# Weight splitting in the second layer of a float32 attention and two-MoE kernel: high parts in two pieces, low parts of five groups on VectorE

## The chip, the cores and the metric

One core of one Trainium2 chip runs the whole kernel. The metric is the device time of one execution in microseconds (us), median of three runs; lower is better. The engines are called TensorE (PE in rows), VectorE (DVE), ScalarE (ACT), GpSimd (POOL) and SyncE (SP), which here only issues DMAs.

## What is computed

The delta-rule attention of 32 heads (4 x 8, 768 steps, head size 48) gives a 3072 x 384 matrix, and two dense layers follow. Only the second of them is touched:

```python
def _moe2_ref(x, w_in, w_out):
    h = x @ w_in                 # 3072 x 384 by 384 x 2048
    r = np.maximum(h, 0.0)
    g = r * r
    return (g @ w_out)           # 2048 x 384
```

## The kernel before

**Precision.** TensorE multiplies numbers of the reduced type float32r. Each float32 tensor is split: the *high* part is a copy by ScalarE that is rounded to float32r, the *low* part is the tensor less its high part. A product takes three matmuls: high by high, high by low, low by high. One matmul here has a 128x128 weight and 512 moving columns; three of them are called a *triple* below.

**Quads.** The second layer works on a pair of 512-token tiles and a group of 256 hidden features (two blocks of 128) at a time. The 2 x 2 result blocks of that *quad* are made with 11 combined products instead of 12 (u, w, c11 twice, t twice, c00, c10 twice, c01 twice), on sums and differences of weights and tokens that are made ahead. There are 3 token pairs and NG = 8 weight groups, so 24 quads: q = 8 * pair + g. The four result blocks b = 0 to 3 pass through ScalarE (relu), VectorE (square), ScalarE (high part, `block_high`) and VectorE (low part, `block_low`), and are then multiplied by `w_out` (`block_output(q, b, kt)`, 12 triples). In TensorE's program the output triples of quad q-1 stand between the products of quad q: 11 + 12 = 23 triples to a quad. Only two PSUM banks hold the products: bank 0 takes u, then c11 on top, then c00, then c01; bank 1 takes w, t, c10. So u of the next quad waits until VectorE has read c01 (`c01_ready`), c11 waits until ScalarE has copied u to `part_u` (`u_part_ready`), t waits for VectorE's `part_w`, c10 for `part_t`, c01 for VectorE's reading of c00.

**Weights of the second layer.** For each group g SyncE loads `w_in` in two DMAs and `w_out` in one into a staging place (`x2_raw` for g from 2 on), GpSimd makes the combinations (`combine_weights`, six instructions), ScalarE makes the high parts (`high_weights`, one instruction of 1280 columns for the `w_in` side, one of 768 for the `w_out` side) and GpSimd the low parts (`low_weights`, 1280 and 768 columns). The load of g+1 waits for both low parts of g, since there is one staging place. Groups 0 to 2 are made during the last tile of the first layer, groups 3 to 7 during quads 0, 1, 2, 4 and 5. Group g is first multiplied in quad g. After group 7, `load_raw(1)` brings the next token pair to the same place, and GpSimd makes five sums (`x2_sums`) and nine low parts (`x2_lows`) of it, ScalarE the nine high parts (`x2_part`), before quad 8; the same again before quad 16.

**What sets the order.** Every engine runs its own program strictly in the written order; semaphores join them. `drain(NTT - 1)` is the copy of the first layer's last accumulators to `y_out`, three ScalarE instructions in quad 0; output triples of block 1 of quad 0 write these accumulators, so they wait for it.

## Time and profile before

| | |
|---|---|
| median of 3 runs | 976.04 us (975.87 to 976.7) |
| the profiled execution | 977.68 us, span of its instructions 975.9 us |
| mean granted TensorE clock | 0.985 |
| TensorE matmul busy | 948.2 us (97%) |
| VectorE busy | 673.8 us (69%) |
| ScalarE busy | 453.9 us (47%) |
| GpSimd busy | 172.4 us (18%) |

Busy shares are unions over the span. Matmuls overlap in the records: one of 512 columns is shown as 0.39 us long, but a new one starts every 0.23 us when nothing holds TensorE up, so a stall is seen in the distance between two starts. The second layer begins at 575.7 us of the span and lasts to its end.

### The profile page before, as it was taken

How to read it: one execution, taken by the hardware profiler on the slowest of the kernel's cores; microseconds unless marked ns; L12 is line 12 of the kernel's file. 1: busy time of each engine (PE TensorE's matmuls, PEld its weight loads, DVE VectorE, ACT ScalarE, POOL GpSimd, SP SyncE). 2: the span in 40 equal slices, each digit the busy share in tenths (PEclk: the TensorE clock that was granted, in tenths of full speed). 3: DMA queues.
4: the chain of work that ended last, by engine and by line, in shares of the span. 5: the costliest groups of instructions: out<-in, count | busy, mean ns of one | idle time of the engine just before them, and what ended most of it. 6: DMA issues, size and time to landing. Idle time of an engine off the chain costs nothing.

```text
span 975.9 us, 23047 instructions
## 1 busy us (share of the span) xinstructions
PE 948.2 (97%) x9448; PEld 767.1 (79%) x9448; DVE 673.8 (69%) x1566; ACT 453.9 (47%) x768; POOL 172.4 (18%) x165
## 2 busy tenths in 40 slices
PE   7899999999999999999999997999999999999997
PEld 6688788778877877787778885787888888888886
DVE  7799798687978788889644545666565564756553
ACT  6667443553355435444545534443453334534333
POOL 5810000000000000000008833543530101400000
PEclk7899999999999999999999998999999999999999
DMA  8252240112012201110013111112002000010001
GB/s 259 83 174 66 60 131 35 34 41 81 35 34 85 69 11 34 48 56 1 2 40 132 52 38 71 39 38 74 29 33 97 1 1 1 6 59 1 1 1 65
DMA packets 31015, 51.71 MB, mean 53 GB/s; under 512 B 2496, under 2 KB 19904, under 8 KB 30912
## 3 DMA queue, kind: packets, MB, share of 16 engines
q1 hardware_dynamic: 30912, 50.24, 15.6%
q8 instruction: 76, 1.25, 0.5%
q14 instruction: 27, 0.22, 0.1%
HBM read 40.80 MB, written 9.44 MB: 51 GB/s over the span
## 4 chain that ended last, share of the span: by engine, by line
PE 83%; DVE 7%; ACT 6%; issue 2%; DMA 2%; SPq 1%; ACTq 0%; DVEq 0%
PE psum L1649 19%; PE psum L1579 18%; PE psum L1569 17%; PE psum L1550 17%; PE psum L1300 2%; PE psum L1386 2%; PE psum L1325 1%; PE psum L1437 1%; DVE act_g L1988 1%; ACT kn_sb L950 1%; PE psum L1444 1%; DMA ring<-in_v_s 1%; PE psum L1251 1%; PE psum L1469 1%; DVE act_g L2032 1%
## 5 line engine op out<-in xcount | busy, mean ns | idle before, releaser
L1579 PE MATMUL psum<-x_high,w 128*128 128x512 f32 x528 | 191.8, 393 | 9.0 <-DVE act_g L2067 6.1
L1569 PE MATMUL psum<-g_hi,w 128*128 128x512 f32 x576 | 197.6, 398 | 0.0
L1550 PE MATMUL psum<-x_hi,w 128*128 128x512 f32 x576 | 197.5, 398 | 0.0
L2032 DVE TENSOR_TENSOR act_g<-act_g 128x512 f32<-128x512 f32 x96 | 75.2, 783 | 82.3 <-ACT act_g L1143 59.1
L1550 PEld LDWEIGHTS psum<-x_hi,w 128*128 128x128 f32 x576 | 108.0, 188 | 26.5
L1569 PEld LDWEIGHTS psum<-g_hi,w 128*128 128x128 f32 x576 | 108.0, 188 | 26.0 <-issue 1.8
L1579 PEld LDWEIGHTS psum<-x_high,w 128*128 128x128 f32 x528 | 100.2, 190 | 31.9 <-issue 10.0
L1569 PE MATMUL psum<-g_lo,w 128*128 128x512 f32 x288 | 112.3, 390 | 0.0
L1550 PE MATMUL psum<-x_lo,w 128*128 128x512 f32 x288 | 111.9, 390 | 0.0
L1046 ACT ACTIVATE act_g<-act_g,half 128x512 f32<-128x512 f32 x86 | 62.2, 723 | 105.3 <-DVE act_g L1984 104.9
L1988 DVE TENSOR_TENSOR act_g<-act_g,psum 128x512 f32<-128x512 f32 x96 | 65.7, 684 | 61.3 <-ACT act_g L1046 57.5
L1649 PE MATMUL psum<-quad_hi,w 128*128 128x512 f32 x288 | 105.6, 396 | 0.0
L1649 PE MATMUL psum<-g_hi,w 128*128 128x512 f32 x288 | 103.8, 389 | 0.0
L1579 PE MATMUL psum<-x_low,w 128*128 128x512 f32 x264 | 103.6, 392 | 0.0
L1054 ACT ACTIVATE g_hi<-act_g 128x512 fp32r<-128x512 f32 x96 | 60.7, 632 | 89.1 <-DVE act_g L1988 60.9
L1993 DVE TENSOR_TENSOR g_lo<-act_g,g_hi 128x512 fp32r<-128x512 f32 x96 | 68.0, 708 | 24.1 <-ACT g_hi L1054 23.0
L1984 DVE TENSOR_SCALAR act_g<-psum 128x512 f32<-128x512 f32 x86 | 58.9, 685 | 21.8 <-PE psum L1550 21.4
L1085 ACT ACTIVATE act_g<-act_g 128x512 f32<-128x512 f32 x72 | 45.6, 633 | 61.1 <-DVE act_g L2058 60.7
L798 POOL TENSOR_TENSOR x_sum<-x_raw 128x512 f32<-128x512 f32 x15 | 20.9, 1412 | 249.6 <-DMA x_raw<-between_layers 162.2
L1649 PEld LDWEIGHTS psum<-quad_hi,w 128*128 128x128 f32 x288 | 55.0, 191 | 12.0 <-issue 0.4
L1649 PEld LDWEIGHTS psum<-g_hi,w 128*128 128x128 f32 x288 | 54.1, 188 | 11.3
L1847 DVE TENSOR_TENSOR x_inv<-x_inv,tmp 128x126 f32<-128x126 f32 (+35 forms) x305 | 62.5, 245 | 0.2
(188 smaller groups left out, 1492.3 us busy)
## 6 DMA issues: line engine op xcount, KB each, us to landing
kt_sb<-in_k_t SPq DMA_DIRECT2D x24, 256.0 KB, 4.1
qt_sb<-in_q_t SPq DMA_DIRECT2D x23, 256.0 KB, 3.4
ring<-in_v_s SPq DMA_DIRECT2D x24, 192.0 KB, 3.1
between_layers<-y_out SPq DMA_DIRECT2D x6, 768.0 KB, 3.5
x_raw<-between_layers SPq DMA_DIRECT2D x6, 768.0 KB, 5.6
gram_or_states<-in_k_s SPq DMA_DIRECT2D x15, 192.0 KB, 2.4
x_raw<-in_w_in SPq DMA_DIRECT2D x6, 384.0 KB, 3.0
x_raw<-in_w_out SPq DMA_DIRECT2D x6, 384.0 KB, 4.1
```

The source lines that it names most:

```text
L1046: act.activation(act_g[n % 2][:, :], act_g[n % 2][:, :], ACT.Square, bias=half[:, 0:1], scale=0.5).then_inc(m_ready, 1)
L1054: act.activation(g_hi[n % 2][:, :], act_g[n % 2][:, :], ACT.Copy).then_inc(g_hi_ready, 1)
L1085: act.activation(quad_act(b)[:, :], quad_act(b)[:, :], ACT.Relu).then_inc(relu_ready, 1)
L1550: ins = pe.matmul(h_ps[n % 2][:, :], w_in_part(f // GW, part)[:, kt, fs], x[:, kt, :], start=(at == 0), stop=(at == len(terms) - 1))
L1569: ins = pe.matmul(acc_ps[0][kt][:, :], w_out_part(f // GW, part)[:, f % GW, ds], g[n % 2][:, :], start=(f == 0 and j == 0), stop=(f == NF ...
L1579: ins = pe.matmul(bank[at][:, :], weight[:, part, w * P:(w + 1) * P], moving[:, x, :], start=(first and c == 0 and j == 0), stop=(c == len ...
L1649: ins = pe.matmul(acc2_of(pair, token_of(b))[kt][:, :], w2[g][:, part, at:at + P], moving[b][:, :], start=(g == 0 and b < 2 and j == 0), s ...
L1847: dve.tensor_tensor(x_inv[:, odd:j + 1:2, j + 1:BLK], x_inv[:, odd:j + 1:2, j + 1:BLK], outer[odd], ALU.add).then_inc(inv_chain, 1)
L1984: dve.tensor_scalar(act_g[n % 2][:, :], h_ps[n % 2][:, :], -1.0, 1.0, ALU.max, ALU.min).then_inc(a_ready, 1)
L1988: dve.tensor_tensor(act_g[n % 2][:, :], act_g[n % 2][:, :], h_ps[n % 2][:, :], ALU.max).then_inc(g_act_ready, 1)
L1993: dve.tensor_tensor(g_lo[n % 2][:, :], act_g[n % 2][:, :], g_hi[n % 2][:, :].bitcast(F32), ALU.subtract).then_inc(g_lo_ready, 1)
L2032: dve.tensor_tensor(quad_act(b)[:, :], quad_act(b)[:, :], quad_act(b)[:, :], ALU.mult).then_inc(square_ready, 1)
```

## The change

The high parts of groups 3 to 7 are no longer made at one place: the 1280-column piece follows `block_high(q, 0)` in quads 0 to 4, the 768-column piece `block_high(q, 1)`. Their low parts are subtracted by VectorE at the end of its quad, groups 3 to 7 in quads 0 to 4; GpSimd keeps groups 0 to 2 and makes only the combinations of the others. The load of `w_in` of the next group no longer waits for the `w_out` side, which has a semaphore of its own. VectorE reads c01 before it squares block 2. TensorE makes one output triple of the old quad before u. `drain(NTT - 1)` moves from behind relu of block 0 to behind `block_high(0, 2)`. The sums for quad 8 each wait for a step of quad 6 or 7.

```diff
             def load_weights2(g):
...
                 elif g:
-                    sp.wait_ge(w2_lo_ready, 2 * g)
+                    sp.wait_ge(w2_lo_ready, 2 * g - 1)
...
+                if g:
+                    sp.wait_ge(w2_lo_ready, 2 * g if g != 2 else 2)
                 sp.dma_start(plain_out(g), w_out2.rearrange("(f p) n -> p f n", p=P)[:, g * GW:(g + 1) * GW, :]
-                             ).then_inc(w2_loaded[at], 16)
+                             ).then_inc(w2_out_loaded[at], 16)
...
                     if pair > 1:
                         pool.wait_ge(w_part_ready, NG * (pair - 1) + i + 3)
+                    elif pair and i == 2:
+                        pool.wait_ge(c01_ready, NG - 1)
+                    elif pair:
+                        pool.wait_ge(w_part_ready, NG - 1 if i < 2 else NG)
...
-            for g in range(1, NG):
+            for g in range(1, EARLY2):
                 combine_weights(g)
                 low_weights(g)
+            for g in range(EARLY2, NG):
+                combine_weights(g)
...
                 act.activation(quad_act(0)[:, :], bank[0][:, :], ACT.Relu).then_inc(relu_ready, 1)
-                if q == 0:
-                    drain(NTT - 1)
                 block_high(q, 0)
...
-                if q in (0, 4):
-                    high_weights(6 if q else 3)
+                if q < NG - EARLY2:
+                    high_weights_in(q + EARLY2)
                 act.wait_ge(c00_ready, q + 1)
                 block_relu(1)
...
                 block_high(q, 1)
-                if q == 5:
-                    high_weights(7)
+                if q < NG - EARLY2:
+                    high_weights_out(q + EARLY2)
...
-                if q == 1:
-                    high_weights(4)
+                if q == 0:
+                    drain(NTT - 1)
                 act.wait_ge(c01_ready, q + 1)
                 block_relu(3)
...
-                if q == 2:
-                    high_weights(5)
...
             def quad(q):
+                block_output(q - 1, 0, 0)
                 if q > 1:
                     u_product(q)
-                block_output(q - 1, 0, 0)
                 block_output(q - 1, 0, 1)
+                if q > 1:
+                    w_product(q)
+                block_output(q - 1, 0, 2)
...
+            def low_weights(g):
+
+                for out_part, cols in enumerate((slice(0, IN_COLS), slice(IN_COLS, ALL_COLS))):
+                    dve.wait_ge(w2_hi_ready, 2 * g + out_part + 1)
+                    dve.wait_ge(w2_lo_ready, 2 * g + out_part)
+                    dve.tensor_tensor(w2[g][:, LOW, cols], staged2(g)[:, cols], w2[g][:, HIGH, cols].bitcast(F32),
+                                      ALU.subtract).then_inc(w2_lo_ready, 1)
...
                 block_low(q, 1)
-                block_square(q, 2)
                 dve.wait_ge(c01_done, q + 1)
                 dve.wait_ge(quad_lo_ready, blocks_by(q, 1))
                 dve.tensor_tensor(quad_act(3)[:, :], part_w[:, :], bank[0][:, :], ALU.subtract).then_inc(c01_ready, 1)
+                block_square(q, 2)
                 block_low(q, 2)
                 block_square(q, 3)
+                if q < NG - EARLY2:
+                    low_weights(q + EARLY2)
```

**VectorE, from the reading of c10 in quad 0 to `part_w` of quad 1.** Line 2062 (later 2090) reads c10, 2067 (2094) reads c01, 2032 (2060) squares, 2037 (2065) is `block_low`, where `g_lo0` and `g_lo1` are blocks 2 and 3, and 2046 (2074) is `part_w`. Before:

```order
L2062 TENSOR_TENSOR act_g0<-part_w,psum 128x512 [waits quad_lo_ready,c10_done]
L2037 TENSOR_TENSOR quad_lo1<-act_g1,quad_hi1 128x512 [waits quad_hi_ready]
L2032 TENSOR_TENSOR act_g0<-act_g0 128x512 [waits relu_ready]
L2067 TENSOR_TENSOR act_g1<-part_w,psum 128x512 [waits quad_lo_ready,c01_done]
L2037 TENSOR_TENSOR g_lo0<-act_g0,g_hi0 128x512 [waits quad_hi_ready]
L2032 TENSOR_TENSOR act_g1<-act_g1 128x512 [waits relu_ready]
L2037 TENSOR_TENSOR g_lo1<-act_g1,g_hi1 128x512 [waits quad_hi_ready]
L2046 TENSOR_TENSOR part_w<-psum,part_u 128x512 [waits c01_ready,u_part_ready,w_done]
```

The same place in the change:

```order
L2090 TENSOR_TENSOR act_g0<-part_w,psum 128x512 [waits quad_lo_ready,c10_done]
L2065 TENSOR_TENSOR quad_lo1<-act_g1,quad_hi1 128x512 [waits quad_hi_ready]
L2094 TENSOR_TENSOR act_g1<-part_w,psum 128x512 [waits quad_lo_ready,c01_done]
L2060 TENSOR_TENSOR act_g0<-act_g0 128x512 [waits relu_ready]
L2065 TENSOR_TENSOR g_lo0<-act_g0,g_hi0 128x512 [waits quad_hi_ready]
L2060 TENSOR_TENSOR act_g1<-act_g1 128x512 [waits relu_ready]
L2055 TENSOR_TENSOR w2_3<-x2_raw,w2_3 128x1280 [waits w2_lo_ready,w2_hi_ready]
L2055 TENSOR_TENSOR w2_3<-x2_raw,w2_3 128x768 [waits w2_lo_ready,w2_hi_ready]
L2065 TENSOR_TENSOR g_lo1<-act_g1,g_hi1 128x512 [waits quad_hi_ready]
L2074 TENSOR_TENSOR part_w<-psum,part_u 128x512 [waits c01_ready,u_part_ready,w_done]
```

The reading of c01 moved ahead of the square of block 2, and two new instructions stand ahead of `block_low` of block 3 and of `part_w`; this is so in quads 0 to 4.

**ScalarE, quad 0 from relu of block 0 to `part_u` of quad 1.** Line 1143 (later 1160) is relu of block 0, 1082 (1098) `block_high`, 1085 (1101) relu of the others, 1062 (1078) the drain, 1132 (1149) `part_u`. Before:

```order
L1143 ACTIVATE act_g0<-psum 128x512 [waits g_lo_ready,c11_done]
L1062 ACTIVATE y_out<-psum 128x512 [waits w_lo_early,w_lo_ready,out_stored,mm2_done]
L1062 ACTIVATE y_out<-psum 128x512 x2
L1082 ACTIVATE quad_hi0<-act_g0 128x512 [waits square_ready]
L1027 ACTIVATE w2_3<-x2_raw 128x1280 [waits mm2_done,w2_combined,w2_loaded1]
L1027 ACTIVATE w2_3<-x2_raw 128x768
L1085 ACTIVATE act_g1<-act_g1 128x512 [waits c00_ready]
L1082 ACTIVATE quad_hi1<-act_g1 128x512 [waits square_ready]
L1085 ACTIVATE act_g0<-act_g0 128x512 [waits c10_ready]
```

In the change, from the high part of block 0 on:

```order
L1098 ACTIVATE quad_hi0<-act_g0 128x512 [waits square_ready]
L1036 ACTIVATE w2_3<-x2_raw 128x1280 [waits mm2_done,w2_combined,w2_loaded1]
L1101 ACTIVATE act_g1<-act_g1 128x512 [waits c00_ready]
L1098 ACTIVATE quad_hi1<-act_g1 128x512 [waits square_ready]
L1042 ACTIVATE w2_3<-x2_raw 128x768 [waits w2_out_loaded1]
L1101 ACTIVATE act_g0<-act_g0 128x512 [waits c10_ready]
L1098 ACTIVATE g_hi0<-act_g0 128x512 [waits square_ready]
L1078 ACTIVATE y_out<-psum 128x512 [waits w_lo_early,w_lo_ready,out_stored,mm2_done]
L1078 ACTIVATE y_out<-psum 128x512 x2
L1101 ACTIVATE act_g1<-act_g1 128x512 [waits c01_ready]
L1098 ACTIVATE g_hi1<-act_g1 128x512 [waits square_ready]
L1149 ACTIVATE part_u<-psum 128x512 [waits w_part_ready,u_done]
```

The drain moved from ahead of the high part of block 0 to ahead of relu of block 3, and the two high pieces of the weights are apart.

**TensorE, the start of quad 2.** The rows that name `w2_2` are u and w of quad 2, those that name `w2_1` are output triples of quad 1. Before:

```order
L1579 MATMUL psum<-x2_high,w2_2 128x512 [waits c01_ready,w2_lo_ready,w2_hi_ready]
L1579 MATMUL psum<-x2_low,w2_2 128x512
L1579 MATMUL psum<-x2_high,w2_2 128x512
L1649 MATMUL psum<-quad_hi0,w2_1 128x512 [waits w2_hi_ready,w2_lo_ready,quad_lo_ready,quad_hi_ready]
L1649 MATMUL psum<-quad_lo0,w2_1 128x512
L1649 MATMUL psum<-quad_hi0,w2_1 128x512 x2
L1649 MATMUL psum<-quad_lo0,w2_1 128x512
L1649 MATMUL psum<-quad_hi0,w2_1 128x512
L1579 MATMUL psum<-x2_high,w2_2 128x512 [waits c10_ready]
```

In the change:

```order
L1662 MATMUL psum<-quad_hi0,w2_1 128x512 [waits w2_hi_ready,w2_lo_ready,quad_lo_ready,quad_hi_ready]
L1662 MATMUL psum<-quad_lo0,w2_1 128x512
L1662 MATMUL psum<-quad_hi0,w2_1 128x512
L1592 MATMUL psum<-x2_high,w2_2 128x512 [waits c01_ready,w2_lo_ready,w2_hi_ready]
L1592 MATMUL psum<-x2_low,w2_2 128x512
L1592 MATMUL psum<-x2_high,w2_2 128x512
L1662 MATMUL psum<-quad_hi0,w2_1 128x512
L1662 MATMUL psum<-quad_lo0,w2_1 128x512
L1662 MATMUL psum<-quad_hi0,w2_1 128x512
L1592 MATMUL psum<-x2_high,w2_2 128x512 [waits c10_ready]
```

The triple u stands one output triple later, and w stays where it was.

## Rows read from the trace of the kernel before

**Rows 1.** Waits of TensorE from 575 us: us in total, times, longest.

```profile
PE psum L1579 <- DVE act_g L2067: 6.1, 3, 3.8
PE psum L1579 <- DVE act_g L2058: 2.2, 1, 2.2
PE psum L1579 <- ACT part_u L1132: 0.6, 1, 0.6
```

**Rows 2.** Stretches: busy us (x count) PE, PEld, DVE, ACT, POOL; clock, DMA.

```profile
575.60:970.20 394.60, 385.59 (x1676) 316.77 (x1674) 228.03 (x314) 161.09 (x265) 82.59 (x65) 0.99 0.08 28
580.00:600.00 20.00, 13.92 (x51) 10.70 (x50) 10.96 (x14) 8.66 (x14) 6.83 (x6) 0.86 0.24 86
680.00:700.00 20.00, 20.00 (x83) 16.34 (x83) 11.64 (x16) 7.71 (x13) 9.35 (x7) 0.92 0.21 79
622.70:626.30 3.60, 3.60 (x17) 2.99 (x16) 2.62 (x4) 1.81 (x3) 3.33 (x6) 1.00 0.02 5
640.00:644.40 4.40, 4.40 (x21) 3.66 (x20) 4.25 (x6) 2.41 (x4) 4.15 (x6) 1.00 0.00 0
```

**Rows 3.** TensorE in order of time: start, length, what, idle before.

```profile
575.71 0.39 PE L1579 MATMUL psum<-x_high,w 128*128 128x512 f32 x1
...
585.68 0.39 PE L1579 MATMUL psum<-x_high,w 128*128 128x512 f32 x1
...
595.14 0.76 PE L1579 MATMUL psum<-x_high,w 128*128 128x512 f32 x1 [3.84 <-DVE act_g L2067]
...
612.30 0.39 PE L1579 MATMUL psum<-x_high,w 128*128 128x512 f32 x1
...
678.43 0.47 PE L1579 MATMUL psum<-x_high,w 128*128 128x512 f32 x1 [2.13 <-DVE act_g L2067]
...
716.66 0.39 PE L1579 MATMUL psum<-x_high,w 128*128 128x512 f32 x1
...
969.75 0.39 PE L1649 MATMUL psum<-g_hi,w 128*128 128x512 f32 x1
```

**Rows 4.** ScalarE in order of time, quad 0.

```profile
580.67 0.60 ACT L1143 ACTIVATE act_g<-psum 128x512 f32<-128x512 f32 x1 [3.48 <-PE psum L1579]
584.75 1.58 ACT L1062 ACTIVATE y_out<-psum 128x512 f32<-128x512 f32 x3 [3.48 <-PE psum L1569]
...
586.72 2.01 ACT L1027 ACTIVATE w<-x_raw 128x1280 fp32r<-128x1280 f32 x2
```

**Rows 5.** VectorE in order of time, quad 0.

```profile
589.28 2.29 DVE L2032 TENSOR_TENSOR act_g<-act_g 128x512 f32<-128x512 f32 x1 [1.12 <-ACT act_g L1085]
...
594.32 0.67 DVE L2067 TENSOR_TENSOR act_g<-part_w,psum 128x512 f32<-128x512 f32 x1
```

**Rows 6.** GpSimd in order of time, quad 0.

```profile
588.08 5.17 POOL L825 TENSOR_TENSOR w<-x_raw,w 128x1280 fp32r<-128x1280 f32 x2 [11.11 <-ACT w L1027]
```

**Rows 7.** Groups by line and shape: count, busy us, mean ns, idle before.

```profile
L825 POOL TENSOR_TENSOR w<-x_raw,w 128x1280 fp32r<-128x1280 f32 x6 | 17.7, 2952 | 43.5 <-ACT w L1027 43.5
...
L1965 DVE TENSOR_TENSOR w<-y_out,w 128x768 fp32r<-128x768 f32 x8 | 7.6, 953 | 1.6 <-ACT w L1000 1.6
L1027 ACT ACTIVATE w<-x_raw 128x1280 fp32r<-128x1280 f32 x6 | 7.6, 1262 | 0.0
...
L1823 DVE TENSOR_TENSOR diag<-diag,ngain 128x1024 f32<-128x1024 f32 x5 | 6.1, 1213 | 0.0
```

**Rows 8.** ScalarE in order of time, quads 7 and 8.

```profile
701.45 0.60 ACT L1143 ACTIVATE act_g<-psum 128x512 f32<-128x512 f32 x1 [2.00 <-PE psum L1579]
...
714.16 0.58 ACT L1132 ACTIVATE part_u<-psum 128x512 f32<-128x512 f32 x1
717.09 0.60 ACT L1143 ACTIVATE act_g<-psum 128x512 f32<-128x512 f32 x1 [2.34 <-PE psum L1579]
```

**Rows 9.** DMA issues from 617 to 627 us: KB each, us to landing.

```profile
x_raw<-in_w_in SPq DMA_DIRECT2D x1, 128.0 KB, 3.3
```

**Rows 10.** VectorE in order of time, low part beside GpSimd's, quad 7.

```profile
704.09 1.78 DVE L2037 TENSOR_TENSOR quad_lo<-act_g,quad_hi 128x512 fp32r<-128x512 f32 x1
```

## What I expect, and why

> **What bounds the kernel now.** I read the waits first, then the windows, then TensorE in order of time with the engine that each stall names. TensorE sets the end: in the second layer it starts its first matmul at 575.71 us and its last at 969.75 [rows 3], and the waits show only five stalls in between, 8.9 us together [rows 1]. The pace of an undisturbed quad is the distance between the relus of block 0 in quads 7 and 8, 717.09 - 701.45 = 15.64 us [rows 8], for 23 triples of three matmuls: 0.68 us a triple, 0.227 us a matmul. The stretch has 1676 matmuls in the windows [rows 2], of which two belong to the step before, so 1673 steps, or 379.3 us at that pace. It took 394.04 us: **14.8 us are lost**, 8.9 as named stalls and 5.9 as slow clock and restarts. The clock: from 580 to 600 us it is 0.86, from 680 to 700 it is 0.92 [rows 2], that is 28% and 16% of 20 us at 1.2 instead of 2.4 GHz, costing 2.8 and 1.6 us; the matmul at 595.14 lasts 0.76 us where one at full clock lasts 0.39 [rows 3]. The last stall ends at 678.43. So all of the 14.8 us lie in quads 0 to 5, the ones that prepare weights.
>
> The reader is to see what is late there. In quad 0 ScalarE does the drain (584.75, 1.58 us) and then both high pieces of group 3 (586.72, 2.01 us) [rows 4] ahead of the work on the blocks. GpSimd then subtracts for 5.17 us from 588.08 [rows 6], and a VectorE square that starts at 589.28 takes 2.29 us instead of 0.69; reading c01 comes behind it, at 594.32 for 0.67 us [rows 5], and u starts at 595.14 after 3.84 us idle [rows 3]. The stall of 2.13 us ahead of 678.43 [rows 3] waits for the same VectorE line.
>
> **The change, part by part.** *GpSimd's low parts of five groups* go: 2.95 us for the first piece [rows 7], 5.17 for both [rows 6], 26 us of work off the path, and with it the long squares. *VectorE gets them.* The 768-column piece has a row of the same operation, 0.953 us; 1280 columns have none. From below 0.953, from above GpSimd's 2.95; 1024 columns take 1.213 [rows 7], which is 0.26 more for 256, so I take 1.48. Together 2.35 us a group, since two in a row overlap by 0.08. They lie behind the square of block 3 and ahead of `block_low` 3 and `part_w`. *The reading of c01* comes earlier by a square, 0.7 us, and *u* later by a triple, 0.68: this wait gains about 1.4 us of room. *ScalarE's pieces*, 1.26 us [rows 7] and 2.01 - 1.26 + 0.08 = 0.83 [rows 4], now fall in its idle time.
>
> **Undisturbed quad, new order** (from the quad's start; each hand-over costs 0.03 us between ScalarE and VectorE, 0.15 from VectorE to TensorE, and a reader starts 0.43 after the product's last matmul starts: 717.09 - 716.66 [rows 3, 8]). c11 starts at 4.08, t at 6.12, c01 ends at 13.6. VectorE reads c01 to 14.5, squares block 2 to 15.1; ScalarE makes its high part to 15.8 and relu 3 to 16.3; square 3 ends at 17.1; low parts of the weights to 19.4; `block_low` 3 to 20.1, `part_w` to 20.7. t of the next quad wants it at 15.64 + 6.12 = 21.76: **0.9 us to spare**. c11 wants `part_u` at 19.72, it is there at 18.3. So five low parts cost nothing in a quad that is on time.
>
> *Are they on time?* Group g+1 runs in a ring: low piece on VectorE 1.48, DMA 3.7 (the second of the pair is issued 0.4 later and lands after 3.3 [rows 9]), GpSimd's six combinations 3.4 (3.33 busy [rows 2]), ScalarE's 1280 columns 1.26, then, since ScalarE takes nothing out of turn, relu 1, square 1, high 1, the 768 columns, relu 2, square 2, high 2, `block_low` 2, square 3 at 0.55 to 0.75 each: 15.75 us, against 15.64 for a quad. Just in balance; a delay once made is not made good by it.
>
> *Quad 0 makes one.* The drain now stands ahead of relu 3. Relu 0 starts at 580.67 [rows 4] and ends at 581.3; square 0 to 582.0, high 0 to 582.65, 1280 columns to 583.8, c00 (its last matmul nine steps ahead of 585.68, at 583.64) read to 584.8, high 1 to 586.8, 768 columns to 587.6, relu 2, square 2, high 2 to 589.5, drain to 591.0, relu 3 591.5, square 3 592.25, high 3 592.9, `part_u` 593.4. TensorE's c10 ends as before (last matmul 585.68 [rows 3]), and c01, no longer held for 2.2 us [rows 1], ends at 587.27. Four triples later it wants the first drained accumulator, at 590.0 (0.06 late), three more later c11, at 592.1: **1.36 us stall** until 593.46. VectorE's low parts run 592.2 to 594.5, `part_w` ends at 595.75, t wants it at 595.6: **0.3**. With three restarts at 0.08, quad 1 loses 1.95. Quad 2 starts at 587.27 + 15.64 + 1.95 = 604.9; before it started at 612.30 [rows 3].
>
> *Quad 2*: the load of group 4 starts at 593.7, its combinations end at 600.8, and relu 1 comes 1 us later than undisturbed; c11 waits 0.27 and t 0.33, 0.76 with restarts. *Quads 3 to 5*: `part_w` at about the moment t wants it, 0.1, 0.25, 0.2. Sum to here 3.25.
>
> *Quads 7 and 8.* The sums now fill GpSimd from `part_w` of quad 7 on, so the first low parts of the tokens run into VectorE's square 1 and `block_low`. Beside such work one `block_low` took 1.78 us instead of 0.69 [rows 10], a square that meets it takes about 1 us more. Before, `part_u` of quad 8 ended at 714.74 [rows 8], and c11 started at 716.66 - 5 x 0.227 = 715.5: 0.8 to spare. The later square 2 takes 1.3 of that and the encounter about 0.8: **1.4 us stall** (0 if nothing meets, 2 at most). Quad 16, where nothing but the order changes, 0.2 (0 to 0.7).
>
> Sum: 14.8 gone, of which I count 14.6 (0.2 us are small steps that stay), less 3.25, 1.4 and 0.2: **-9.7 us**. The profiled execution took 977.68 us, span 975.9; the median is 976.04, so I take the difference off the median: 966.3.
>
> **Rivals.** *Clock:* stalls of 1.36 and 0.3 in quad 1 bring TensorE to 1.2 GHz, as 2.2 and 3.84 did (2.8 us) or 2.13 (1.6): 968 to 969. For it: 2.13 was enough once; against: 2.2 alone was not, the granted clock fell only behind the 3.84. [...]
>
> *The ring is longer than the quad:* the combinations took 4.15 us beside a busy VectorE at 640 us [rows 2] instead of 3.33; with a slower load too, 1 us a quad over four quads: 970.3.
>
> *All hidden:* the rows of quad 0 are early by the 1.4 us that I count late, and nothing meets in quad 8; about 1.1 us stays: 962.5.
>
> *VectorE and GpSimd meet:* the long square that started at 589.28 ended 0.5 us after GpSimd's piece of 2.95 (588.08 + 2.95 = 591.03) [rows 5, 6, 7], so it waited for all of it. If the new VectorE pieces held GpSimd's combinations up in the same way, the ring would be 2.35 us longer, 2.4 us a quad in quads 2 to 5, and the gain gone: 976. Against it: the combinations of g+1 wait for a load that is issued only behind the first piece of g and takes 3.7, while the second takes 0.95. The Trainium skill, "SBUF — State Buffer", section "SBUF: two separate sides", says that a VectorE operation with two SBUF inputs and a GpSimd one take turns, whole instruction by whole instruction; the trace agrees, and by the rule the hold cuts both ways.
>
> *Slower than before:* VectorE takes as long for the pieces as GpSimd did, 5.17 instead of 2.35 us. `part_w` is then late by 2.8 us in every quad once quad 1 has used the spare 0.9, five times 2.8 = 14 us, and the clock falls at least once, 1.6: 966.3 + 14 + 1.6 = 982. It decides from 9.7 / 5 = 1.9 us more a group on. The 768-column row speaks against it.
>
> **How the numbers follow.** Main case 0.55 (its own range 963.5 to 968.2), clock 0.15, ring 0.17, all hidden 0.06, slower 0.04, VectorE and GpSimd meet (no change) 0.03. A measurement of this kernel tells 0.2% from nothing, 2 us. Main, clock, ring and hidden give faster, 0.93. The range takes in main, clock and ring: 963.0 to 970.8.
>
> **What would show it.** Right: no VectorE square over 1.8 us in quads 0 to 6; VectorE rows of 128x1280 at about 1.48; TensorE waits for `part_u` about 1.4 us in quad 1 and again in quad 8, for `part_w` under 1 us in all; quad 2 starting near 605. Wrong: a wait of ScalarE's 1280-column piece for GpSimd that grows from quad to quad, a wait of t over 1 us in each of quads 2 to 5, or a granted clock below 1 in quads 1 to 3.

## The result and the profile after

The changed kernel takes **972.85 us** (median of 7 runs, 971.66 to 973.5) beside 977.14 for the kernel before on the same chip (7 runs, 975.87 to 979.32): a ratio of **0.9957, 95% interval 0.9945 to 0.9969**. It is faster, by 4.3 us. I forecast 9.7 us and 966.3, with a range that ended at 970.8: the sign is right and the size is not.

The profiled execution took 973.39 us with a span of 971.0. Its page, span and busy times:

```profile
span 971.0 us, 23057 instructions
PE 948.7 (98%) x9448; PEld 764.0 (79%) x9448; DVE 671.1 (69%) x1576; ACT 450.6 (46%) x768; POOL 147.4 (15%) x155
```

TensorE is as busy as before, GpSimd has lost 25 us, and VectorE, which got ten instructions more, is busy for less time than before (673.8): it no longer stands waiting inside its own squares.

The waits of TensorE from 575 us on, us in total, times, longest (answers to [rows 1]):

```profile
PE psum L1592 <- ACT part_u L1149: 1.3, 2, 1.0
PE psum L1662 <- ACT y_out L1093: 1.2, 2, 0.6
PE psum L1592 <- DVE part_w L2074: 0.9, 5, 0.2
PE psum L1592 <- DVE act_g L2094: 0.5, 1, 0.5
PE psum L1662 <- ACT x_sum L1093: 0.3, 2, 0.2
```

Five waits of 8.9 us together became twelve of 4.2. The waits of 3.8 and 2.1 us for the reading of c01 and the one of 2.2 us for the reading of c00 (L2058 before) are gone, as forecast. The second row from above and the last, on L1662, which is an output triple, stand nowhere in the prediction.

The stretches (columns as in [rows 2]):

```profile
576.70:965.60 388.90, 384.57 (x1676) 312.61 (x1674) 226.00 (x324) 157.72 (x265) 55.66 (x52) 1.00 0.08 28
580.00:600.00 20.00, 18.77 (x81) 14.57 (x80) 13.43 (x19) 9.87 (x16) 1.39 (x3) 1.00 0.25 86
```

The clock of the second layer is 1.00: no slow stretch is left, where 580 to 600 us had 0.86 before. TensorE in order of time (answers to [rows 3]):

```profile
576.79 0.39 PE L1592 MATMUL psum<-x_high,w 128*128 128x512 f32 x1
...
594.59 0.50 PE L1592 MATMUL psum<-x_high,w 128*128 128x512 f32 x1 [0.95 <-ACT part_u L1149]
597.11 0.50 PE L1592 MATMUL psum<-x_high,w 128*128 128x512 f32 x1 [0.19 <-DVE part_w L2074]
607.44 0.47 PE L1592 MATMUL psum<-x_high,w 128*128 128x512 f32 x1 [0.50 <-DVE act_g L2094]
613.61 0.50 PE L1592 MATMUL psum<-x_high,w 128*128 128x512 f32 x1 [0.18 <-DVE part_w L2074]
...
720.73 0.47 PE L1662 MATMUL psum<-quad_hi,w 128*128 128x512 f32 x1 [0.58 <-ACT y_out L1093]
```

The last matmul starts at 965.15, so the second layer took 388.4 us from first to last start, against 394.04, and its loss over the undisturbed 379.3 is **9.1 us where I forecast 5.05** (3.25 + 1.4 + 0.2, and 0.2 of small steps). A stall costs more than its idle time, since the matmuls ahead of it run out and start up again; so I add up, around each stall, what the distance of two starts exceeds 0.227 us by:

| place | forecast | measured |
|---|---|---|
| quad 1 (accumulator, c11, t) | 1.95 | 2.03 |
| u of quad 2 | 0 | 0.74 |
| quad 2, c11 and t | 0.76 | 0.73 |
| quads 3 to 5 | 0.55 | 2.11 |
| quad 8, c11 | 1.4 | 0.54 |
| quads 9 and 17, output triples | 0 | 2.50 |
| quad 16 | 0.2 | 0 |
| small steps (what is left of 9.07) | 0.2 | 0.42 |

That is 4.0 us more than forecast. The rest between the two profiled executions lies outside my sum: the second layer starts 1.1 us later (576.79 against 575.71, with the same program ahead of it), what follows the last matmul is 0.3 us shorter, and 0.6 us more lies outside the span. -9.7 + 4.0 + 1.1 - 0.3 + 0.6 = -4.3, which is 973.39 - 977.68.

**Where the ring was late.** GpSimd's first combination of groups 4 to 7 starts when the load has landed; three of these rows, and the combinations of group 4 after its first two:

```profile
598.61 0.46 POOL L820 TENSOR_TENSOR x_raw<-x_raw 128x128 f32<-128x128 f32 x1 [23.61 <-DMA x_raw<-in_w_in]
...
599.45 0.96 POOL L822 TENSOR_TENSOR x_raw<-x_raw 128x128 f32<-128x128 f32 x1
600.38 1.17 POOL L823 TENSOR_SCALAR x_raw<-x_raw 128x384 f32<-128x384 f32 x1
...
615.09 0.46 POOL L820 TENSOR_TENSOR x_raw<-x_raw 128x128 f32<-128x128 f32 x1 [12.58 <-DMA x_raw<-in_w_in]
631.57 0.47 POOL L820 TENSOR_TENSOR x_raw<-x_raw 128x128 f32<-128x128 f32 x1 [12.56 <-DMA x_raw<-in_w_in]
```

ScalarE, which stood waiting for the last of these combinations, and what came behind it on ScalarE:

```profile
602.59 1.27 ACT L1036 ACTIVATE w<-x_raw 128x1280 fp32r<-128x1280 f32 x1 [4.27 <-POOL x_raw L827]
603.77 0.61 ACT L1101 ACTIVATE act_g<-act_g 128x512 f32<-128x512 f32 x1
```

And VectorE beside them, and its two new instructions of one group:

```profile
599.40 0.69 DVE L2065 TENSOR_TENSOR quad_lo<-act_g,quad_hi 128x512 fp32r<-128x512 f32 x1
```

```profile
L2055 DVE TENSOR_TENSOR w<-x_raw,w 128x1280 fp32r<-128x1280 f32 x5 | 7.4, 1485 | 0.0
L2055 DVE TENSOR_TENSOR w<-x_raw,w 128x768 fp32r<-128x768 f32 x5 | 4.8, 959 | 0.5
```

The ring takes 16.48 us (615.09 - 598.61, and again 631.57 - 615.09) where I had 15.75 and a quad takes 15.64. Its subtraction is as forecast, 1.485 against 1.48. The combinations last from 598.61 to 602.51, 3.9 us instead of 3.4: the third is held until VectorE's `block_low` of 599.40 is over, 0.96 us instead of 0.46. In the other three groups they take 3.8 to 3.9 us too. The load takes 3.8 instead of 3.7. And ScalarE does nothing for 4.27 us while relu of block 1, whose input has been there since 600.87, stands behind the weights' piece. This wait of ScalarE is 4.27, 4.28, 4.18 and 4.10 us for groups 4 to 7: it does not grow from quad to quad, the sign that I had named for a late ring, since each quad is held back together with the ring.

**Where the prediction had no step.** ScalarE at the end of quad 8:

```profile
719.47 0.63 ACT L1098 ACTIVATE g_hi<-act_g 128x512 fp32r<-128x512 f32 x1 [2.01 <-DVE act_g L2060]
720.00 1.55 ACT L1093 ACTIVATE y_out<-psum 128x512 f32<-128x512 f32 x3
721.43 0.64 ACT L1101 ACTIVATE act_g<-act_g 128x512 f32<-128x512 f32 x1
```

`drain2` copies the accumulators of the token pair that is over; the first output triple of the next quad writes the first of them. The copies stand behind the high part of block 2, which now waits for a later square, and the output triple moved one place earlier, ahead of u. So at 720.73 TensorE waits for the first copy, and shortly behind for the next, in quad 9 and again in quad 17.

### The profile page after: what moved, and what is told of

It is laid out like the page before. It is cut to its first block, busy times and chain, and to the rows that moved or that the text cites. A ratio compares the mean times of both kernels' runs of the same rounds, so it can differ in the third digit from the quotient of the medians.

```text
span 971.0 us, 23057 instructions
## 1 busy us (share of the span) xinstructions
PE 948.7 (98%) x9448; PEld 764.0 (79%) x9448; DVE 671.1 (69%) x1576; ACT 450.6 (46%) x768; POOL 147.4 (15%) x155
## 4 chain that ended last, share of the span: by engine, by line
PE 76%; DVE 9%; ACT 7%; issue 3%; DMA 3%; POOL 1%; SPq 1%; ACTq 0%; DVEq 0%
PE psum L1582 17%; PE psum L1563 17%; PE psum L1662 15%; PE psum L1592 15%; PE psum L1313 2%; PE psum L1399 2%; DVE act_g L2060 2%; PE psum L1338 1%; PE psum L1450 1%; DVE act_g L2008 1%; ACT kn_sb L960 1%; PE psum L1457 1%; DMA x_raw<-in_w_in 1%; PE psum L1264 1%; PE psum L1482 1%
## 5 line engine op out<-in xcount | busy, mean ns | idle before, releaser
L2060 DVE TENSOR_TENSOR act_g<-act_g 128x512 f32<-128x512 f32 x96 | 68.2, 711 | 76.5 <-ACT act_g L1160 46.7
L1662 PE MATMUL psum<-quad_hi,w 128*128 128x512 f32 x288 | 108.2, 391 | 1.6 <-ACT y_out L1093 1.2
L1662 PE MATMUL psum<-g_hi,w 128*128 128x512 f32 x288 | 103.8, 389 | 0.0
L1662 PEld LDWEIGHTS psum<-quad_hi,w 128*128 128x128 f32 x288 | 54.0, 188 | 14.8 <-ACT g_hi L1098 2.0
L1662 PEld LDWEIGHTS psum<-g_hi,w 128*128 128x128 f32 x288 | 54.1, 188 | 11.3
L1863 DVE TENSOR_TENSOR tmp<-diag,x_inv 128x126 f32<-128x126 f32 (+35 forms) x305 | 62.4, 245 | 0.3
```

Of the source, the lines that this page charges most:

```text
L1662: ins = pe.matmul(acc2_of(pair, token_of(b))[kt][:, :], w2[g][:, part, at:at + P], moving[b][:, :], start=(g == 0 and b < 2 and j == 0), s ...
L1863: dve.tensor_tensor(outer[odd], scaled_diag(n)[:, j:j + 1, j + 1:BLK].to_broadcast(part), x_inv[:, odd:j + 1:2, j:j + 1].to_broadcast(part ...
L2060: dve.tensor_tensor(quad_act(b)[:, :], quad_act(b)[:, :], quad_act(b)[:, :], ALU.mult).then_inc(square_ready, 1)
```

## The experiments

Theories: **Swap**, the swap carries the gain (long squares go) and the change's other edits give part of it back at three places: the ring, the drain of quad 0, the copies of quads 8 and 16. **Work**, VectorE's new work in the middle of each quad is what is dear. **Order**, the order of the other edits brings a gain by itself. (The expectations use the letters A, B and C for theories of their own, new in each run.) Ratios are to the kernel before, run beside each, with 95% intervals; "loss" is the second layer's length from first to last matmul start, less 379.3 us, in the profiled execution (before 14.7).

**The change again.** 

> The change as it is, once more beside the kernel before, as the reference for the three kernels that follow on the same chip. Ratio near 0.9957. The trace of the change starts the second layer 1.07 us later than that of before, and most of that (0.9 us) is already there at 55 us, where both programs are the same. If that is chance in TensorE's clock at the start, this trace starts the second layer at another time, within 1 us of 575.7; if the change causes it, again at 576.8.

974.49 us, ratio 0.9964 (0.9951 to 0.9978), loss 9.9: u of quad 2 lost 1.3 us instead of 0.7. This median is 1.6 us above the first one and the second layer 0.8 us longer, so differences below are good to about 1 us by the second layer and 1.6 by the medians, and most are given both ways.

**Without the swap.** GpSimd subtracts all low parts again; every other edit stays.

```diff
             for g in range(EARLY2, NG):
                 combine_weights(g)
+                low_weights(g)
...
                 block_square(q, 3)
-                if q < NG - EARLY2:
-                    low_weights(q + EARLY2)
```

> The change with the low parts of groups 3 to 7 back on GpSimd, everything else as in the change. Theory A (the ring load, combinations, 1280 columns on ScalarE, blocks, low piece on VectorE is longer than a quad, since ScalarE waits for the combinations with relu 1 behind it): the ring leaves the blocks out and is about 12 us, so the combinations are early again in quads 2 to 5, but squares of 1.3 to 2.3 us come back; quads 2 to 5 lose about 0.3 us each instead of 0.7, quad 1 loses more; in all 0 to 1.5 us faster than the change. Theory B (VectorE has simply too much to do and is late with part_w): all waits of TensorE in quads 2 to 5 go, 3 us or more faster than the change. Theory C (the long squares are what costs): 3 us or more slower than the change.

977.04 us, **0.9998 (0.9989 to 1.0006)**, loss 13.9. Nothing is left of the gain, and the long squares are back: 2.6 us slower than the change by the medians, 4.0 to 4.8 by the second layer. So of the expectation's own theories it is C, the long squares, and not A, which had this run 0 to 1.5 us faster. GpSimd's subtraction, then VectorE in order of time:

```profile
605.64 2.92 POOL L833 TENSOR_TENSOR w<-x_raw,w 128x1280 fp32r<-128x1280 f32 x1 [1.44 <-ACT w L1037]
606.11 3.00 DVE L2061 TENSOR_TENSOR act_g<-act_g 128x512 f32<-128x512 f32 x1 [4.41 <-ACT act_g L1102]
...
610.61 0.69 DVE L2095 TENSOR_TENSOR act_g<-part_w,psum 128x512 f32<-128x512 f32 x1
611.21 1.75 DVE L2061 TENSOR_TENSOR act_g<-act_g 128x512 f32<-128x512 f32 x1
```

The waits of TensorE, first row:

```profile
PE psum L1593 <- DVE act_g L2095: 3.9, 2, 3.7
```

The square of 3.00 us is followed by a wait of 3.7 us for the reading of c01. **Order** falls: the new orders alone bring nothing.

**Only the swap.** On the kernel before, the low parts of groups 3 to 7 go to VectorE at the end of quads 0, 1, 2, 4 and 5, where their high parts are made; no order is touched.

```diff
-            for g in range(1, NG):
+            for g in range(1, 3):
                 combine_weights(g)
                 low_weights(g)
+            for g in range(3, NG):
+                combine_weights(g)
...
                 block_square(q, 3)
+                if q in (0, 1, 2, 4, 5):
+                    low_weights({0: 3, 1: 4, 2: 5, 4: 6, 5: 7}[q])
```

> The kernel before with one part of the change alone: VectorE subtracts the low parts of groups 3 to 7, at the end of quads 0, 1, 2, 4 and 5; high parts, loads, drain, TensorE's order as before. The long squares (2.3 us) go, and with them the slow clock: of the 12 to 15 us that before loses, the stall of 2.2 us behind the drain of quad 0 stays, the others shrink. If the swap of engines carries the gain of the change, 3 to 6 us faster than before; if it needs the two pieces and the new orders, less than 2.

970.51 us, **0.9917 (0.9903 to 0.9932)**, loss 6.0: 7 us, more than the whole change brings. Its waits, all of them, and the matmul behind the longer:

```profile
PE psum L1581 <- DVE act_g L2068: 2.2, 1, 2.2
PE psum L1581 <- DVE act_g L2077: 0.6, 1, 0.6
```

```profile
589.95 0.77 PE L1581 MATMUL psum<-x_high,w 128*128 128x512 f32 x1 [2.24 <-DVE act_g L2068]
```

The first half of **Swap** holds; the runs that follow are on the second. What is left is the wait for the reading of c00, late by way of the drain ahead of the high part of block 0, with a clock of 0.91 from 580 to 600 us. The change removes this wait, and its other edits bring small ones that cost 9.1 us with their restarts.

**The weights' first piece later.** The 1280 columns stand directly ahead of the 768, behind `block_high` 1, so that relu of block 1 no longer stands behind the combinations.

```diff
                 block_high(q, 0)
-                if q < NG - EARLY2:
-                    high_weights_in(q + EARLY2)
...
                 block_high(q, 1)
                 if q < NG - EARLY2:
+                    high_weights_in(q + EARLY2)
                     high_weights_out(q + EARLY2)
```

> The change with ScalarE's 1280-column piece moved from ahead of relu 1 to behind the high part of block 1, directly ahead of the 768-column piece. Theory A: relu 1, square 1 and high 1 no longer stand behind the combinations, the ring falls below 15.6 us, and the waits of quads 2 to 5 (2.9 us in all) nearly go: 2.3 to 3.2 us faster than the change. Theory B (VectorE has too much to do): VectorE's work is the same, within 0.5 us of the change.

970.0 us, 0.9924 (0.9911 to 0.9937), loss 6.2: by the medians 4.5 us below the change run beside it, by the second layer 3.7 (2.9 against the first profile of the change). No wait is left in quads 2 to 5. The first combinations of three groups:

```profile
614.47 0.47 POOL L820 TENSOR_TENSOR x_raw<-x_raw 128x128 f32<-128x128 f32 x1 [10.98 <-DMA x_raw<-in_w_in]
629.79 0.46 POOL L820 TENSOR_TENSOR x_raw<-x_raw 128x128 f32<-128x128 f32 x1 [11.46 <-DMA x_raw<-in_w_in]
645.22 0.46 POOL L820 TENSOR_TENSOR x_raw<-x_raw 128x128 f32<-128x128 f32 x1 [11.58 <-DMA x_raw<-in_w_in]
```

15.3 and 15.4 us apart instead of 16.5, shorter than a quad: the ring now catches up. VectorE has the same work as in the change, so **Work** falls as the cause of these waits. The price is 1.0 us in quad 1, where the drained accumulator comes later.

**The copies of quads 8 and 16 earlier.** They stand ahead of the high part of block 2.

```diff
-                block_high(q, 2)
                 if g == 0 and pair:
                     drain2(pair - 1, 0)
+                block_high(q, 2)
```

> The change with the copy of the finished accumulators in quads 8 and 16 moved ahead of the high part of block 2. If the waits of TensorE for y_out at 720.73 and 847.17 come from this copy standing behind a high part that the new order of the squares makes 1.3 us later, they go (2 x 0.82 us), and those for x_sum four triples on (2 x 0.4) shrink too: 1.6 to 2.5 us faster than the change. If the copy waits for something else (the store of the place, TensorE itself), no difference.

970.48 us, 0.9927 (0.9914 to 0.994), loss 6.7: 4.0 us by the medians, 3.2 and 2.4 by the second layers, the latter what I expected. The rows for `y_out` and `x_sum` are gone from the waits; one of 0.3 us for GpSimd's `x_low` is new.

**The square of block 2 back** ahead of the reading of c01, but in quads 5 to 23 alone.

```diff
                 block_low(q, 1)
+                if q >= NG - EARLY2:
+                    block_square(q, 2)
...
-                block_square(q, 2)
+                if not (q >= NG - EARLY2):
+                    block_square(q, 2)
```

> The change with VectorE's square of block 2 back ahead of the reading of c01 in quads 5 to 23, where no weights are made. If the new order makes the copies of quads 8 and 16 late, the high part of block 2 comes 1.3 us earlier and the waits for y_out and x_sum go: 1.5 to 2.4 us faster than the change, and u has enough room (it stands a triple later), so no new wait for the reading of c01. If u needs the new order, waits for VectorE's c01 line come in quads 6 to 23, up to 0.3 us each.

969.68 us, 0.9922 (0.991 to 0.9934), loss 6.0, 3.1 less than the change. The waits of quads 8, 9 and 17 are gone and no new one has come: without the later square none of the three is there.

**The drain of quad 0 in three single copies**, behind relu 1, 2 and 3, in place of one block of 1.55 us.

```diff
                 block_relu(2)
+                if q == 0:
+                    drain_one(1)
...
-                if q == 0:
-                    drain(NTT - 1)
```

> The change with the three drain copies of quad 0 apart: behind relu 1, relu 2 and relu 3, each in an idle stretch of ScalarE, instead of all three ahead of relu 3. If the drain there is what makes part_u of quad 1 late (1.1 us stall) and the first drained accumulator too (0.25), both go, 1.4 us and two restarts. What of it stays at the end tells of the ring: if quads 2 to 5 are bound by it, an earlier start of quad 1 is kept only as far as relu 3 and the low piece of group 3 come earlier, 1.4 us; so 1.2 to 2 us faster than the change. If the drain is harmless, no difference.

970.98 us, 0.9937 (0.9924 to 0.9949), loss 7.6, 1.5 less than the change. `part_u` waits 0.3 us in all where it waited 1.3; quads 2 to 5 lose 3.3 us where they lost 3.6.

**VectorE subtracts the 1280 columns twice,** in the change, so its cost there is measured by itself.

```diff
+                    if out_part == 0:
+                        dve.tensor_tensor(w2[g][:, LOW, cols], staged2(g)[:, cols], w2[g][:, HIGH, cols].bitcast(F32),
+                                          ALU.subtract).then_inc(first_time, 1)
+                        dve.wait_ge(first_time, g - EARLY2 + 1)
                     dve.tensor_tensor(w2[g][:, LOW, cols], ...
```

> The change with VectorE's 1280-column low piece made twice for each of groups 3 to 7 (the same values, the second time in front of the semaphore), 1.55 us more a group. Theory A (the ring is longer than a quad, 16.5 against 15.64 us): there is no spare time, so each of the five pieces costs its full length: 7 to 8 us slower than the change. Theory B (each quad has 0.9 us to spare at part_w, as predicted): (1.55 - 0.9) x 4 + 1.55, about 4 us slower.

980.48 us, 1.0031 (1.0021 to 1.004), loss 17.0: 7.6 us above the change by the medians, 8.0 by the second layer, about 1.5 for each of five waits for `part_w`. The row of its waits, and the stretch of its second layer:

```profile
PE psum L1593 <- DVE part_w L2079: 8.5, 5, 1.7
```

```profile
575.70:972.00 396.30, 384.23 (x1674) 312.56 (x1673) 233.04 (x329) 157.27 (x264) 55.69 (x52) 1.00 0.08 28
```

In the change each quad from 1 to 5 is late already, so each us more on VectorE there costs a full us.

**The same double subtraction with the later first piece**, where quads 2 to 5 are on time. The edit is that of both runs above.

> The same doubling in the kernel with ScalarE's 1280-column piece moved next to the 768-column piece. There the ring is off the path and part_w has spare time again: quad 1, which has a wait for part_w already, pays 1.55, quads 2 to 5 about 0.75 each: 3.5 to 5 us slower than without the doubling (970.0). If it costs 7 to 8 us as well, the moved piece did not free the ring.

977.01 us, 0.9994 (0.9984 to 1.0003), loss 12.9; 7.0 us above the run with the later piece alone, 6.7 by the second layer. I expected 3.5 to 5. Quad 1 pays 1.5, quads 2 to 5 pay 1.1 to 1.2 each: of the added 1.5 us the spare takes 0.4, not 0.9. It isn't the ring that waits here: GpSimd's last combination of a group, and ScalarE's piece behind it without idle time between it and `block_high` 1:

```profile
621.08 0.46 POOL L828 TENSOR_TENSOR x_raw<-x_raw 128x128 f32<-128x128 f32 x1
```

```profile
622.13 0.63 ACT L1099 ACTIVATE quad_hi<-act_g 128x512 fp32r<-128x512 f32 x1 [0.76 <-DVE act_g L2064]
622.66 1.26 ACT L1037 ACTIVATE w<-x_raw 128x1280 fp32r<-128x1280 f32 x1
```

The combinations are done at 621.54, 1.1 us ahead of the piece. So it is the spare at `part_w`. But the later piece has itself used half of that spare. Relu of block 2 stands behind it and behind the 768 columns, and VectorE, which is through with the reading of c01, stands idle for 0.43 us ahead of the square of block 2:

```profile
624.56 0.62 ACT L1102 ACTIVATE act_g<-act_g 128x512 f32<-128x512 f32 x1
625.21 0.69 DVE L2064 TENSOR_TENSOR act_g<-act_g 128x512 f32<-128x512 f32 x1 [0.43 <-ACT act_g L1102]
```

The same 0.43 us stands in quad 3 of the run with the later piece alone, where `part_w` ends 0.48 us before t starts in quad 4, 0.33 without the hand-over of 0.15. My estimate for a timely quad in the change's own order is therefore 0.33 + 0.43, or 0.8 us, near the 0.9 of the prediction. No run shows it: in the change all five quads behind a weight subtraction are late. The expectation of 3.5 to 5 us carried the 0.9 over into an order in which it is not there.

**The three mendings together**: the later piece (quads 1 to 4), single copies of the drain, the earlier copies of quads 8 and 16.

> The change with three edits together: in quads 1 to 4 the 1280-column piece directly ahead of the 768-column piece, the copies of quads 8 and 16 ahead of the high part of block 2, and the three drain copies of quad 0 apart. If the three losses are separate and additive, of the 9.1 us that the second layer loses about 1 us is left (the wait at c11 of quad 8, 0.5, and small ones): 7 to 8.5 us faster than the change, 0.987 to 0.989 of before. If one hides behind another, less.

965.03 us, **0.9875 (0.986 to 0.9891)**, loss 1.35. Waits of 0.3 and 0.2 us, once each, are all that is left.

**And the square back in quads 5 to 23.**

> The three edits together and, in addition, VectorE's square of block 2 ahead of the reading of c01 in quads 5 to 23. The only stall left behind quad 1 is the one at c11 of quad 8, 0.47 us; it went with this order in the run that tried it alone. 0.5 to 0.7 us faster than the three edits together (965.0); if their drain copies ahead of the high part cost something now, nothing.

964.63 us, **0.9859 (0.9845 to 0.9874)**, loss 0.8, a single wait of 0.2 us. Its second layer is 0.54 us shorter than with the three edits, as expected; the medians, 0.4 us apart, do not tell the two from each other. It is 13 us below the kernel before.

**The kernel before, one more profile.** 

> The kernel before once more for its trace. The four programs with low parts on VectorE start the second layer at 576.6 to 577.1 us, before and the one with them on GpSimd at 575.7 and 575.8; at 35 to 38 us the same six matmuls take 3.3 us in the first and 2.6 in the second. By chance of the clock, this trace may show either; by cause, 575.7 again.

976.37 us, loss 12.5, the second layer from 576.66 to 968.45. The same waits stand there, the longest of them 2.3 us instead of 3.8: the profile I worked from showed 2.2 us more to be gained in the second layer than this one.

## Why the prediction was only half right

**The bound and the mechanism: right.** GpSimd's subtractions held VectorE's squares, the squares held the reading of c01, and that held u. Moving the subtraction takes this away: 7 us by itself in the run with only the swap, and the change without the swap is no faster than the kernel before. No square in quads 0 to 6 is long any more.

**VectorE's price: right.** 1.48 forecast, 1.485 measured; 0.953 and 0.959 for the second piece. The case "slower" fell with it. The double subtraction shows what it would have cost.

**Quad 1 and the start of quad 2: right.** 1.95 forecast, 2.03 measured, at the three places named (accumulator 0.33 for 0.14, c11 1.24 for 1.44, t 0.46 for 0.38). Quad 2 starts with its first output triple, at 606.1, which is 29.3 us behind the second layer's first matmul; forecast 604.9 - 575.71 = 29.2. Quad 2's c11 and t: 0.76 forecast, 0.73 measured.

**The ring, the term that failed in size.** "15.75 us, against 15.64 for a quad. Just in balance". It takes 16.48, 0.73 more. The step that failed is "GpSimd's six combinations 3.4"; they take 3.9, which is 0.5 of the 0.73. The 3.4 comes from a stretch in which VectorE was busy for 2.62 of 3.60 us [rows 2], but there GpSimd's instructions came first and VectorE's had to wait, a square for 0.82 and a `block_low` for 0.94 us instead of 0.69; in the change `block_low` came first, and GpSimd waited. The load takes 0.1 more, and another 0.1 is the square of block 2, which waits behind the reading of c01 (it starts at 607.21, relu of block 2 ends at 607.02): an order that the change itself brings and that my ring left out. One half of "VectorE and GpSimd meet" thus happened: not with the new subtractions, which don't fall together with the combinations, as I argued, but with the old low part of block 0. I had priced the same lengthening in the rival "the ring is longer than the quad" (970.3, at 1 us a quad); it came at 0.7 a quad. The Trainium skill, "SBUF — State Buffer", section "SBUF: two separate sides", which I cited there, says that whichever of the two instructions starts first is served whole and the other waits for its end. The trace agrees in both directions: 0.46 became 0.96 on GpSimd here, and 0.69 became 3.00 on VectorE without the swap, behind a subtraction of 2.92 us.

One more thing made it dear. u of quad 2 waited 0.5 us, since relu 1 behind the weights' piece makes the whole chain of the quad late, up to the reading of c01; I followed only c11 and t. Quads 2 to 5 thus lost 3.6 us where I had 1.3. The run with the later piece shows the place: its combinations still take 3.85 us (614.47 to 618.32), but with relu 1 ahead of them the ring is 15.3 to 15.4 and all waits in these quads are gone.

**Quads 9 and 17, a step left out.** For the later square 2 I asked who waits for `part_u`, and not who else stands behind the high part of block 2. `drain2` stands there, and the output triple that needs it had itself been moved earlier. 2.5 us in all. Both the run that moves the copies and the run that moves the square back take it away.

**Quad 8, an encounter counted twice.** It cost 0.54 us where I had 1.4. The 0.8 us between `part_u` and c11 came from quad 8 of the kernel before, and VectorE's long instructions beside GpSimd's low parts of the tokens were already in it. The square of block 3 ahead of that `part_u` before, and the square of block 2 in the same quad of the change:

```profile
711.81 1.78 DVE L2032 TENSOR_TENSOR act_g<-act_g 128x512 f32<-128x512 f32 x1
```

```profile
703.43 1.29 DVE L2060 TENSOR_TENSOR act_g<-act_g 128x512 f32<-128x512 f32 x1
```

In quads 10 to 15, where no tokens are prepared, `part_u` ends 2.6 us before c11 starts in the kernel before and 1.5 us in the change: the new order takes 1.1 us, not 1.3. The preparation of the tokens, these encounters and ScalarE's high parts together, takes 1.8 us of it in quad 8 of the kernel before (2.6 - 0.8) and again 1.8 in the change (`part_u` ends at 708.19, 0.3 us behind the place of an undisturbed c11). To a row that had the encounters I added 0.8 for them once more. Quads 8, 9, 16 and 17 together cost 3.0 for 1.6.

**The clock, right to leave out.** The granted clock of the second layer is 1.00 in the change, where the longest wait is 0.95 us, and in the run with the double subtraction, with five waits of 1.7 us; a wait of 1.9 us without the swap left it at 1.00 too (590 to 596 us). Longer waits went either way, which my "2.2 alone was not" did not know: it rests on one profile. Behind the wait of 2.24 us in quad 0 of the kernel before, the first profile and the second:

```profile
588.30:592.00 3.70, 2.98 (x12) 2.16 (x12) 2.72 (x2) 1.34 (x3) 3.70 (x2) 1.00 0.19 80
```

```profile
589.20:592.40 3.20, 3.14 (x8) 2.52 (x9) 2.17 (x1) 1.00 (x2) 3.20 (x2) 0.50 0.23 94
```

Behind the wait of 2.1 us near 678 us it is the other way round, 0.65 (678.4 to 682.4) in the first and 1.00 (678.2 to 682.2) in the second. What decides between the two, the runs do not show. With only the swap, the clock was 0.91 from 580 to 600 us, around a wait of 2.24 us.

**One profile as the base.** I took the difference off one profiled execution and the median of another three runs. Beside the change the kernel before had 977.14, 1.1 us more than the median I started from, and the second profile of it has 2.2 us less to lose in the second layer but starts it 1.0 us later. These are not errors of a step, but they belong in the range: 4.5 us above the forecast were too few for a base that moves by 1 us and a ring without spare.

## What to carry to other kernels

When work moves to another in-order engine, list everything that now stands behind each moved or delayed instruction and who waits for it, on the places outside the steady pattern too (here the first quad of each token pair). A ring of load, combine, round and subtract whose sum comes out within 1% of the period has no room for a single instruction that meets another (here 15.75 us became 16.48): either move the waiting instruction behind the work that is ready (2.9 to 3.7 us here), or count the excess for every round. Before an order is changed together with an assignment, run each alone: here the assignment gave 7 us, the orders around it took 2 to 4 back, and with four small mendings all of it came to 13. And a spare that is read from a row already holds what happened there: look at the same distance in an undisturbed place before anything is added to it.

## What the runs showed of the hardware that was not expected

**VectorE holds GpSimd as well.** A combination of 128 columns takes 0.46 us, and 0.96 when it meets `block_low`, an operation of two SBUF inputs of 0.69 us.

**The start of the second layer moves by 1.7 us between executions** whose programs up to there do the same, from 575.67 (double subtraction) to 577.35 us: 575.71 and 576.66 in two profiles of the kernel before, 576.79 and 577.10 in two of the change, 577.35 with only the swap. It arises early; the stretch from 30 to 40 us in three profiles, in this order: the kernel before, its second profile, only the swap.

```profile
30.00:40.00 10.00, 9.37 (x178) 6.94 (x178) 8.67 (x41) 5.63 (x14) 5.77 (x14) 0.83 0.02 7
```

```profile
30.00:40.00 10.00, 9.31 (x144) 7.13 (x144) 7.92 (x40) 4.87 (x11) 5.83 (x15) 0.70 0.01 3
```

```profile
30.00:40.00 10.00, 8.64 (x142) 6.86 (x142) 7.03 (x38) 4.76 (x11) 5.67 (x14) 0.65 0.02 5
```

The granted clock differs, 0.83, 0.70 and 0.65, and TensorE gets through 178, 144 and 142 matmuls in the same 10 us. Over all 14 profiles the matmuls go with the start better than the clock does: the six with 175 to 178 in this stretch start the second layer at 575.67 to 576.28 us, the eight with 142 to 151 at 576.28 to 577.35, and one of the eight (copies of quads 8 and 16 earlier) has 144 at a clock of 0.83. What makes the difference stays open; a single profile of this kernel carries about 1 us of it.
